# The one-token level of later tiles computed with tokens as rows, and the weights' low parts written at other times

## Time and profile before

| what | us |
|---|---|
| median of 3 runs | 1038.78 (1038.64 to 1040.95) |
| the profiled execution | 1038.0 |
| its span in the profile | 1036.2 |
| PE busy in the span | 1000.8 (97%) |
| DVE busy | 486.2 (47%) |
| ACT busy | 467.9 (45%) |
| POOL busy | 427.7 (41%) |

### The profile page before, as it was taken

One profiled execution on the slowest core, in us unless ns is written; L12 is line 12 of the kernel. 1 busy time (PEld: TensorE's weight loads), 2 busy tenths in 40 slices (PEclk: granted clock), 3 DMA queues, 4 the chain that ended last, 5 costly groups with the idle time before them and its releaser, 6 DMA issues.

```text
span 1036.2 us, 19675 instructions
## 1 busy us (share of the span) xinstructions
PE 1000.8 (97%) x8151; PEld 832.0 (80%) x8151; DVE 486.2 (47%) x614; ACT 467.9 (45%) x848; POOL 427.7 (41%) x360
## 2 busy tenths in 40 slices
PE   4797899999999999999999999999999999999997
PEld 4686688888888888888888888888888888888886
DVE  7779747844854775495356422223222222232221
ACT  5764657658666765867355322222222222221211
POOL 7768634752764575275256211211122112211221
PEclk9998999999999999999999999999999999999999
DMA  9531015005003301300531010010100100000000
GB/s 360 211 127 62 1 50 206 2 13 213 32 2 115 141 2 40 126 32 2 184 124 61 1 62 0 1 62 1 45 17 1 61 1 1 31 1 0 31 1 31
DMA packets 17369, 63.53 MB, mean 61 GB/s; under 512 B 1920, under 2 KB 2176, under 8 KB 16512
## 3 DMA queue, kind: packets, MB, share of 16 engines
q1 hardware_dynamic: 17280, 62.27, 16.6%
HBM read 52.82 MB, written 9.44 MB: 60 GB/s over the span
## 4 chain that ended last, share of the span: by engine, by line
PE 89%; DVE 3%; issue 3%; POOL 3%; DMA 1%; ACT 0%; SPq 0%; POOLq 0%; ACTq 0%; DVEq 0%
PE acc L539 11%; PE acc L541 11%; PE acc L540 11%; PE bank L565 7%; PE bank L567 7%; PE bank L566 7%; PE hid L525 6%; PE hid L527 6%; PE hid L526 6%; PE bank L389 5%; PE hid L565 2%; PE hid L567 2%; PE hid L566 2%; DVE scores L894 2%; PE bank L446 1%
## 5 line engine op out<-in xcount | busy, mean ns | idle before, releaser
L1082 POOL TENSOR_TENSOR g_lo<-prod,g_hi 128x512 fp32r<-128x512 f32 x72 | 93.0, 1292 | 347.5 <-ACT g_hi L775 347.5
L1075 POOL TENSOR_TENSOR g_lo<-act_tmp,g_hi 128x512 fp32r<-128x512 f32 x96 | 128.5, 1339 | 173.2 <-ACT g_hi L736 173.2
L977 DVE TENSOR_TENSOR sig<-sig,bank 128x512 f32<-128x512 f32 x72 | 49.5, 688 | 275.4 <-ACT sig L769 275.4
L775 ACT CAST g_hi<-prod 128x512 fp32r<-128x512 f32 x72 | 44.7, 621 | 248.1 <-PE acc L541 248.1
L1040 POOL TENSOR_TENSOR keys<-keys,gates 128x512 f32<-128x512 f32 x82 | 108.8, 1328 | 73.2 <-PE bank L389 47.0
L525 PE MATMUL hid<-x_hi,win_hi 128*128 128x512 f32 (+1 forms) x297 | 118.9, 400 | 6.3 <-DVE act_tmp L965 6.3
L539 PE MATMUL acc<-g_hi,wout_hi 128*128 128x512 f32 x288 | 115.2, 400 | 2.1 <-POOL g_lo L1075 2.1
L527 PE MATMUL hid<-x_hi,win_lo 128*128 128x512 f32 (+1 forms) x297 | 115.3, 388 | 0.0
L526 PE MATMUL hid<-x_lo,win_hi 128*128 128x512 f32 (+1 forms) x297 | 115.2, 388 | 0.0
L540 PE MATMUL acc<-g_lo,wout_hi 128*128 128x512 f32 x288 | 112.8, 392 | 0.0
L541 PE MATMUL acc<-g_hi,wout_lo 128*128 128x512 f32 x288 | 112.7, 391 | 0.0
(11 more groups left out here) (90 smaller groups left out, 1869.1 us busy)
## 6 DMA issues: line engine op xcount, KB each, us to landing
gates<-in_f_dram SPq DMA_DIRECT2D x12, 512.0 KB, 5.5
queries<-in_q_dram SPq DMA_DIRECT2D x12, 512.0 KB, 4.9
keys<-in_k_dram SPq DMA_DIRECT2D x12, 512.0 KB, 4.8
values<-in_v_tok_dram SPq DMA_DIRECT2D x6, 1024.0 KB, 7.9
q_tok<-in_q_tok_dram SPq DMA_DIRECT2D x12, 384.0 KB, 8.2
k_tok<-in_k_tok_dram SPq DMA_DIRECT2D x12, 384.0 KB, 8.7
x_dram<-x_out SPq DMA_DIRECT2D x6, 768.0 KB, 3.2
x_raw<-x_dram SPq DMA_DIRECT2D x6, 768.0 KB, 5.6
```

Of the source, the lines that this page charges most:

```text
L1075: pool.tensor_tensor(g_lo[:, c % RING, :], act_tmp[:, 2 + c % 2, :], g_hi[:, c % RING, :].bitcast(F32), ALU.subtract).then_inc(g_lo_done, 1)
```

## The change

- From unit 2 on (`APART = 2`) the level of one token is no longer two steps of PE, two copies of ACT and two takes from PSUM. Instead a query's gate and the query of the next token are loaded with tokens as rows (`load_next_gates`, `load_next_queries`, both into `q_tok`), ACT takes the sigmoid (`next_gate`), POOL multiplies the keys by it (`next_key`), DVE multiplies by the next token's query (`next_own`), reduces (`next_sum`) into `nexts`, and writes that into `scores` with the mask of the one-token level (`place_nexts`). All but the last stand in negative slots. `scale_q`, `scale_k` and `merge` of the level stay, at slots 0 and 1.
- Gates, diagonal placing and first gating of units 2 to 5 get other slots.
- In the first two units the products with the identity (line 441) use 32 columns of weights each, 12 for a batch, where there were 3 of 128 columns.
- Unit 0: `own_first` and `sum_own` stand two slots later, and `own_first(0)` waits until POOL has done 12 steps of `scale_k`; `take_last` is split by halves of the heads, and the outputs of batches 0 and 1 wait for the first half alone; `hidden` of the first chunk runs in two groups of 256 columns, not four of 128.
- Low parts: the last four of w_in move from chunks 1 to 4 into the head (POOL); two of w_out stand in the head on DVE (one before), the others at chunks 0, 1, 2, 9, 11 and 13 (before: 1, 2, 4, 6, 7, 8, 9). Five casts of w_out and the last of w_in stand on ACT in the head.
- Unit 1: `own`, `sum_own` and `own_value` move from slots 3 to 13 to slots 9 to 20.
- `copy_right` comes ahead of `take_blocks`, `take_whole` and `take_last` on ACT within a slot.
- The last chunk: the products with g_hi run before g_lo is waited for; the result leaves in three stores of 256 KB, copied by ACT, DVE and ACT (`project_last`, `store_last`), not one of 768 KB.

```diff
-FIRST = Plan(own=(), diag=(18, 20), own_v=(21, 22), place=(), sigmoid=(-6, -5), gated=(-6, -4),
+FIRST = Plan(own=(), diag=(20, 22), next_gate=(), next_key=(), next_own=(), next_sum=(),
+             own_v=(21, 23), place=(), sigmoid=(-6, -5), gated=(-6, -4),
...
-    p = Plan(own=(-13, -12), diag=(-11, -10), own_v=(), place=(-9, -8, -6, -4), sigmoid=(-2, -1), gated=(-1, 0),
+    p = Plan(own=(-13, -12), diag=(-11, -10), own_v=(), next_gate=(-9, -8), next_key=(-8, -7), next_own=(-5, -4), next_sum=(-4, -3),
+             place=(-5, -3, 0, 1), sigmoid=(-2, -1), gated=(-1, 0),
...
-SECOND = usual((6, 9, 12, 14, 16), 18, 21, 23, own=(3, 5), diag=(8, 10), own_v=(11, 13), place=(), sigmoid=(-2, -1),
-               gated=(-1, 1))
-USUAL = usual((2, 5, 8, 11, 13), 16, 19, 21)
-PLANS = [FIRST, SECOND, USUAL._replace(place=(-8, -7, -5, -4))] + [USUAL] * (UNITS - 3)
-
-
-W2_SLOTS = (1, 3, 5, 6, 7, 8)
+SECOND = usual((6, 9, 12, 14, 16), 18, 21, 23, own=(9, 11), diag=(17, 18), own_v=(19, 20), place=(), sigmoid=(-2, -1),
+               gated=(-1, 1), next_gate=(), next_key=(), next_own=(), next_sum=())
+USUAL = usual((2, 5, 8, 11, 13), 16, 19, 21, sigmoid=(-3, -2), gated=(-2, 0))
+USUAL = USUAL._replace(take=[2, 4] + USUAL.take[2:], scale=[0, 1] + USUAL.scale[2:], turn=[0, 1] + USUAL.turn[2:])
+PLANS = [FIRST, SECOND, USUAL._replace(own=(-11, -10), diag=(-9, -8), next_gate=(-7, -6), next_key=(-6, -5), next_own=(-4, -3), next_sum=(-3, -2))] + [USUAL] * (UNITS - 3)
...
-W2_SLOTS = (1, 3, 5, 6, 7, 8)
+W2_EARLY = 5
+W2_SLOTS = (8, 10, 12)
...
+def apart(a):
+    return 2 if a >= APART else 0
...
-    return a * FILLS + i
+    return a * FILLS + max(i, apart(a)) - sum(apart(b) for b in range(a + 1))
...
+            if a > APART:
+                sp.wait_ge(next_done, 2 * (a - APART))
...
+        def load_next_gates(a):
+            for g in range(2):
+                sp.wait_ge(diag_done, 2 * a + g + 1)
+                sp.dma_start(tok_group(q_tok, g), tok_group(fn[a], g)).then_inc(fn_in[g], 16)
+        def load_next_queries(a):
+            for g in range(2):
+                sp.wait_ge(next_keyed, 2 * (a - APART) + g + 1)
+                sp.dma_start(tok_group(q_tok, g), tok_group(qn[a], g)).then_inc(qn_in[g], 16)
...
+        def store_last():
+            for dm in range(KC):
+                sp.wait_ge(sum_took[dm], 1)
+                sp.dma_start(out[UNITS - 1][:, dm], result[:, dm, :]).then_inc(stored, 16)
...
         for a in range(1, UNITS):
+            if a >= APART:
+                load_next_gates(a)
             load_q(a)
             if a == 1:
                 load_f(a)
             load_k(a)
+            if a >= APART:
+                load_next_queries(a)
             if a > 1:
                 load_f(a)
...
+            if a == 0 and b == 0:
+                pe.wait_ge(half_took, 1)
+            if b == (2 if a == 0 else 0):
+                pe.wait_ge(act_took, a * ACT_A_UNIT + ACT_Y)
...
-                for kc in range(KC):
-                    v = own_values[:, b * DM + kc * P:b * DM + (kc + 1) * P]
-                    pe.matmul(of(a, i)[:, kc * P:(kc + 1) * P], v, eye[:, :], start=(kc == 0), stop=False)
+                for p in range(PAIRS):
+                    for t in range(3):
+                        c = b * DM + Q * (3 * p + t)
+                        pe.matmul(place(p, t), own_values[:, c:c + Q], eye[:, :], start=(3 * p + t < 4), stop=False)
...
-                level(a, s)
+                if s >= apart(a):
+                    level(a, s)
...
-            for b in range(B if n == 0 else 1):
-                t = slice(b * P, (b + 1) * P) if n == 0 else slice(0, UT)
+            for g in range(2 if n == 0 else 1):
+                t = slice(2 * g * P, 2 * (g + 1) * P) if n == 0 else slice(0, UT)
                 if c == 0:
-                    pe.wait_ge(x_hi_done, m * B + (b + 1 if n == 0 else B))
-                    pe.wait_ge(x_lo_done, m * B + (b + 1 if n == 0 else B))
...
+        def project_last(c):
+            n = chunk2(UNITS - 1, c)
+            pe.wait_ge(g_hi_done, n + 1)
+            for dm in range(KC):
+                for part in range(2):
+                    w = wo[c // 2][part][:, c % 2, dm * P:(dm + 1) * P]
+                    pe.matmul(acc[dm][:, :], w, g_hi[:, c % RING], start=False, stop=False)
+            pe.wait_ge(g_lo_done, n + 1)
+            for dm in range(KC):
+                w = wo[c // 2][0][:, c % 2, dm * P:(dm + 1) * P]
+                pe.matmul(acc[dm][:, :], w, g_lo[:, c % RING], start=False, stop=True).then_inc(sum_done, 1)
...
+        def next_gate(a, g):
+            act.wait_ge(fn_in[g], 16 * (a - APART + 1))
+            t = tok_group(q_tok, g)
+            act.activation(t, t, ACT.Sigmoid).then_inc(next_gates, 1)
...
+        def take_last_first(g):
+            act.wait_ge(filled, fill(0, Y0))
+            act.wait_ge(dve_took, MASKED)
+            for e in range(2):
+                t = bank[fill(0, LAST0 + e) % 3]
+                for par in range(2):
+                    last = act.copy(group(scores, g)[rows(0), par::2, e, HALF:P],
+                                    t[rows(par), g * BP // 4 * HALF:(g + 1) * BP // 4 * HALF
+                                      ].rearrange("p (x t) -> p x t", t=HALF))
+                if g == 1:
+                    last.then_inc(act_took, 1)
+            if g == 0:
+                last.then_inc(half_took, 1)
...
+                if a == 0:
+                    split_w2(b)
...
-            if h in (26, 28):
-                split_w2((h - 26) // 2)
-            if h == 29:
+            if h == 26:
...
+            if g == 0:
+                dve.wait_ge(k_scaled, COPIES)
...
+        def next_own(a, g):
+            dve.wait_ge(qn_in[g], 16 * (a - APART + 1))
+            dve.wait_ge(next_keyed, 2 * (a - APART) + g + 1)
+            t = tok_group(q_tok, g)
+            dve.tensor_tensor(t, t, tok_group(k_tok, g), ALU.mult).then_inc(next_owned, 1)
+        def next_sum(a, g):
+            dve.wait_ge(next_owned, 2 * (a - APART) + g + 1)
+            dve.tensor_reduce(nexts[:, g * BP:(g + 1) * BP], tok_group(q_tok, g).rearrange("p (x d) -> p x d", d=D),
+                              AXIS_X, ALU.add).then_inc(next_done, 1)
+        def place_nexts(a, g):
+            dve.wait_ge(next_done, 2 * (a - APART) + g + 1)
+            dve.wait_ge(diag_placed, B * (a - PLAIN) + 2 * (g + 1))
+            for half in range(2):
+                o = group(scores, g)[rows(half), :, :, half * HALF:(half + 1) * HALF]
+                o = o.rearrange("p x e (b s r) -> p (x e) b s r", s=2, r=1)[:, :, :, 1, :]
+                i = nexts[rows(half), g * BP:(g + 1) * BP].rearrange("p (x b r) -> p x b r", b=1, r=1)
+                last = dve.copy_predicated(o, level_mask(0, half), i.broadcast_to([HALF, BP, HALF // 2, 1]))
...
+                if s < apart(a):
+                    place_nexts(a, s)
+                else:
+                    take_level(a, s)
...
-                split_w2(0)
+                for i in range(2):
+                    split_w2(i)
...
-                if m == 0 and c == 1:
-                    split_w2(1)
+                if m == 0 and c < W2_EARLY - 2:
+                    split_w2(c + 2)
                 if m == 0 and c - 1 in W2_SLOTS:
-                    split_w2(2 + W2_SLOTS.index(c - 1))
+                    split_w2(W2_EARLY + W2_SLOTS.index(c - 1))
...
+        def next_key(a, g):
+            pool.wait_ge(next_gates, 2 * (a - APART) + g + 1)
+            t = tok_group(k_tok, g)
+            pool.tensor_tensor(t, t, tok_group(q_tok, g), ALU.mult).then_inc(next_keyed, 1)
...
-            elif 25 <= h < 28:
-                split_w1(h - 24)
+            elif 24 <= h < 24 + W1N - 1:
+                split_w1(h - 23)
...
-                if m == 0 and 1 <= c < W1N - 3:
-                    split_w1(c + 3)
```

More of the change, by code:

```diff
@@ L35 @@
 RING = 2
+APART = 2
 W1N, W2N = FC1 // 2, FC1 // 2
@@ L65 @@
 H_FIRST = -13
-Plan = namedtuple("Plan", "own diag own_v place sigmoid gated copy step take block_take scale turn whole whole_take last last_take "
+Plan = namedtuple("Plan", "own diag own_v next_gate next_key next_own next_sum place sigmoid gated copy step take block_take scale turn whole whole_take last last_take "
                           "decay y y_out tk tk_out kv state state_place")
-FIRST = Plan(own=(), diag=(18, 20), own_v=(21, 22), place=(), sigmoid=(-6, -5), gated=(-6, -4),
+FIRST = Plan(own=(), diag=(20, 22), next_gate=(), next_key=(), next_own=(), next_sum=(),
+             own_v=(21, 23), place=(), sigmoid=(-6, -5), gated=(-6, -4),
              copy=(-6, -4, 1, 3, 5, 7, 9, 11, 13, 15, 17, 19), step=(0, 2, 4, 6, 8, 10, 12, 14, 16, 18),
@@ L114, in turns, with copied @@
     return now
+def apart(a):
+    return 2 if a >= APART else 0
 def fill(a, i):
-    return a * FILLS + i
+    return a * FILLS + max(i, apart(a)) - sum(apart(b) for b in range(a + 1))
+def copied(a, n):
```

(13 more changed lines are left out.)

69 lines of the change are left out of this document (48 added, 21 removed).

## The result

The kernel after takes 1048.24 us (median of 4 runs, 1047.78 to 1049.54) against 1038.71 for the kernel before beside it: ratio 1.0089, 95% interval 1.0073 to 1.0105. It is slower by 9.5 us where the prediction had 1020.0 us, in a range of 1011 to 1028. The profiled execution took 1048.58 us, its span 1046.8.

The account below looks back on a forecast made before the run. PE, busy 97%, was taken as the bound, with DVE bounding 75 to 100 us. Terms -8.1 - 13.4 + 5.5 - 0.9 - 1.8 = -18.7 from 1038.0 gave 1019.3, the median 1020 us, range 1011 to 1028.

Parts of the forecast that it names:

- I take 0 for all this: Units 2 to 5: the replacing work on ACT, POOL and DVE and the added loads were to cost 0 us.
- It fits, barely: Slots -4 to 5: DVE's 17 to 18.2 us of work were to fit in PE's 18.4 us.
- Levels left out of PE: Units 2 to 5: one pair of PE steps fewer each, 4 x 2.02 = -8.1 us.
- DVE stays the bound: Rival: placing, next_own and next_sum held up 1 us each beside POOL; PE loses 8 us, 1028; chance 0.12.
- The slower rival: Units 2 to 5: gates' loads 4.7 us late in each unit, then half clock; 32 us, 1052; chance 0.03.
- The chunks of unit 0: Unit 0's chunks: DVE work moved out leaves 3 us of 16.4 lost to PE's waits, -13.4 us.
- outputs of unit 1: Unit 1's four batches of outputs fall from 0.87 to 0.66 us each, -0.9 us.
- The head: Up to hidden(2): late diag_done delays loads, sigmoids wait, clock halves; +5.5 us (between +2 and +8).
- the loads are in time: Rival: loads don't delay the head, which gives -2.9 and not +5.5 us, 1011.6; chance 0.2.
- The tail: Last chunk: g_hi's products first 0.4, two engines copying 0.9, a smaller last store 0.5; -1.8 us.

Follow-up runs that it names:

- y3: Kernel after with all levels of units 2 to 5 on PE again, their diagonal, sigmoids, first gating and scaling at old slots; 1030.02 us (0.9902).
- n1: Kernel after with the one-token level of units 2 to 5 left out altogether, its loads and replacing work too; 1023.66 us (0.9843).
- s1: x2 with next_own at slots 15 and 16 and next_sum at 16 and 17, behind the levels; 1026.76 us (0.9874).
- x2: Kernel after with place_nexts cut to an operation on one column, so the level is not written; loads, products, sums stay; 1034.85 us (0.9951).
- x3: Kernel after with place_nexts reading a PSUM bank in place of nexts, so the written values are wrong; 1034.30 us (0.9951).
- y2: Kernel after with next_sum writing into spare columns of a PSUM bank and place_nexts reading them there; 1034.57 us (0.9957).
- s3: y2 with the one-token level of unit 2 left on PE (APART = 3) and x1's order of loads; 1030.70 us (0.9911).
- x1: Kernel after with unit 1's q_tok and k_tok loaded behind its queries and gates; 1048.26 us (1.0086).
- r1: Kernel after with next_own, next_sum and the placing at slots 13 to 16, behind the levels, the placing waiting for ACT; 1061.39 us.
- r2: Kernel after with the placing alone moved behind the levels, to slots 15 and 16, waiting for ACT; 1056.66 us.

## Why the prediction was wrong

- **The step that failed** is the sum's first term, "I take 0 for all this", with its ground "It fits, barely". Levels left out of PE: forecast -8.1, measured +18.2 (1048.24 less y3's 1030.02). By differences of medians it is made of -6.4 for PE's steps (n1), +3.1 for the loads, sigmoids, key products and sums behind the levels (s1), +8.1 for having the products and sums before slot 0 (x2), and +13.4 for the placing (after). The profiles from `hidden(2)` on, without the head and its spread, give -5.2, +1.9, +5.6 and +13.7, together +16.0. Of the four only the second is as small as the noise.
- **The placing was priced from the wrong row.** The earlier trace rows gave 1.02 as the mean of all levels' takes. The one-token level's take, which `place_nexts` resembles, was 1.36 in the trace of before, so even without POOL beside it (1.3 us) the placing took next to nothing off DVE; with both inputs in SBUF beside POOL it is 1.98; and the cost that decides is neither, but that g_lo beside it goes from 1.29 to 2.16. On DVE the 16 placings take 29.7 us where the forecast had 16.3; PE's waits for g_lo grew by 15.3.
- **The rival "DVE stays the bound" named this mechanism and was given 0.12 and 8 us.** Its price counted DVE's delay and left out POOL's, and it trusted that POOL had little to do in those slots; g_lo is there in every chunk, and `scale_k` had been moved to slots 0 and 1, beside the placing. x2, x3 and y2 show the mechanism by 14 us: 2.16 against 1.29 us on POOL and 1.98 against 1.33 on DVE with both inputs in SBUF, and 1.29 and 1.33 in y2 with one in PSUM. The rule of the Trainium skill (SBUF — State Buffer, Who interferes with whom), that a DVE instruction with two SBUF inputs and a GpSimd instruction that reads SBUF contend, and that with at most one SBUF input they don't, agrees with both, here for a predicated copy.
- **"It fits, barely" had no room for a wait.** The sum of 17 to 18.2 us of work in 18.4 counted no idle time, yet DVE waited for q_next's load (2.1 us in unit 2, 3.89 in x2) and for the sigmoids (2.5 in unit 4) with `activate` queued behind. The first wait reached PE in x2 and y2. The second is about as long in units 3 to 5 of n1 (2.35), where PE waits 0.3 us a unit, so there it isn't shown to cost anything. The slower rival had `load_f` late in every unit and took 32 us for it; in unit 2 alone something of the kind is seen, 1.50 us of PE's in s1, beside the late `q_next`. Unit 2 held about 4 us of y2's loss (s3); how much of that is the late load and how much DVE's work was not parted.
- **The chunks of unit 0** were right: with the outputs of unit 1 forecast -14.3, measured -12.7, and PE's waits for `activate` there went from 6.3 to 0.4 us. y3, with the level on PE, was to give -10.6 by the forecast's other terms and gave -9.4.
- **The head**: the chain through `diag_done`, the loads, the sigmoids and the clock was as said, and its size too small in this profile, +8.95 for +5.5; eleven other profiles of the same order of work had +4.4 to +9.0. The first load went out 3.4 us later than forecast, which is the whole difference: `own_first` began at 43.22 and not 41.8, the first own values took 2.10 and not 1.02, the second `own_first` 2.58 and not 1.5. What the forecast did not have is PE's wait of 3.42 us for batch 2's own values; it was hidden here behind the later gates. But it makes the price of the rival "the loads are in time" wrong: with the gates in time (x1), `hidden(2)` started 3.0 us later than before, not 2.9 earlier.
- **The tail**: -1.8 forecast, -1.6 measured.
- PE's period without any replacing work, from unit 3 to unit 4, fell by 1.54 us (89.59 to 88.05) and not 2.02: in n1 PE still waits for g_lo, 0.9 us in unit 2 and 0.3 in each of units 3 to 5. `gated` and `scale_q` (both inputs in SBUF) lie beside a subtraction of 2.14 us there, at their new slots; that they are the reason is argued, not tested.
- Open: why the clock fell in x1's units 3 and 4 and not in the kernel after's, how the rest of s1's 3.1 us divides (1.8 of them lie in unit 2, behind the late gates), and how much of what s1 gave back in unit 2 is the wait for the load.

## What to carry to other kernels

Before work is moved from the bounding engine to one "with room", price it from the row of its own form, not from a group's mean over several forms, and ask what the engine beside it does then: here a DVE instruction with both inputs in SBUF also lengthened POOL's (1.29 to 2.16 us), and POOL's subtraction fed PE in every chunk. One operand kept in PSUM undid all that the placing cost. An instruction that waits for a load or another engine costs its wait to whatever is queued behind it, so it belongs behind what the bounding engine waits for (here `activate`), and a move that needs a new wait (r1, r2) can cost more than the crowding that it avoids.

## What the runs showed of the hardware

- The predicated copy of 64x512 has two lengths by its pattern: 1.33 to 1.36 us for the one- and two-token levels, 0.72 to 0.74 for the levels of 4, 8 and 16 tokens. The first is about 1.3 whether the data come from PSUM (y2, median 1329 ns) or from SBUF with POOL mostly idle (r2, median 1302 ns); from SBUF beside POOL the median was 1980 ns.
- A `tensor_reduce` of 128x768 took 0.94 to 0.95 us in every place, beside POOL too, and as much with its output in PSUM.
- After a wait of PE of about 3.5 us the granted clock fell to about half, in the head (0.50 in 68 to 72 us) as in the steady units (0.54 in r2); after the waits of 0.6 to 2.2 us in units 3 and 4 of the kernel after it stayed at 1.00, while behind the 2.19 us wait in unit 2, and behind waits of the same length in units 2 to 4 of x1, it was 0.72 over 6 us. So equal waits had either outcome.
